# Attention: reciprocal row sums stored to DRAM, read back spread over feature rows, and multiplied into the PV output

## What is computed

```python
# q, k, v: (4, 8, 576, 64); block-causal mask in blocks of 64
scores = scale * q @ k.T
scores = where(block_i >= block_j, scores, -1e9)
attn = exp(scores - max(scores))
attn = attn / (sum(attn) + 1e-9)
out = attn @ v            # -> x (2304, 512), into the gated FFN and the experts
```

## Time and profile before

| | us |
|---|---|
| median of 3 runs (lowest, highest) | 1021.81 (1020.45, 1022.78) |
| profiled execution, its own time | 1020.62 |
| its span, first to last instruction | 1018.8 |
| attention, last PV's end in the span | 245.9 |
| TensorE busy in the span | 947.3 (93%) |
| VectorE busy in the span | 386.7 (38%) |
| mean granted TensorE clock | 0.970 |

### The profile page before, as it was taken

One profiled execution on the slowest core, in us unless ns is written; L12 is line 12 of the kernel. 1 busy time (PEld: TensorE's weight loads), 2 busy tenths in 40 slices (PEclk: granted clock), 3 DMA queues, 4 the chain that ended last, 5 costly groups with the idle time before them and its releaser, 6 DMA issues.

```text
span 1018.8 us, 15358 instructions
## 1 busy us (share of the span) xinstructions
PE 947.3 (93%) x5050; PEld 783.1 (77%) x5051; DVE 386.7 (38%) x962; ACT 341.1 (33%) x774; POOL 244.9 (24%) x241
## 2 busy tenths in 40 slices
PE   6898889988999999999999999999578998999995
PEld 3554545556999999999999999999457887888884
DVE  6878777784221120120111011011654444225421
ACT  4656666664222111211211211211254344125310
POOL 2122122121121111111111111111163545215511
PEclk9999999998999999999999999999679999999998
DMA  4234434331211010010010000000265538115310
GB/s 124 70 104 124 124 89 124 112 120 56 83 44 41 32 32 1 32 32 1 32 32 1 32 1 1 32 1 1 112 225 179 202 127 268 41 51 206 118 41 29
DMA packets 57313, 78.28 MB, mean 77 GB/s; under 512 B 22703, under 2 KB 34991, under 8 KB 57264
## 3 DMA queue, kind: packets, MB, share of 16 engines
q1 hardware_dynamic: 51504, 62.42, 19.7%
q0 software_dynamic: 3360, 10.49, 3.0%
q10 hardware_dynamic: 2400, 4.72, 1.2%
HBM read 63.46 MB, written 14.68 MB: 77 GB/s over the span
## 4 chain that ended last, share of the span: by engine, by line
PE 82%; DVE 7%; issue 6%; POOL 2%; DMA 2%; ACT 0%; SPq 0%; POOLq 0%; DVEq 0%; ACTq 0%
PE bank L1153 21%; PE bank L1155 21%; PE bank L1154 21%; PE bank L1084 6%; PE bank L1121 5%; PE bank L1103 3%; DVE prob L814 3%; PE bank L1290 2%; PE bank L1212 1%; DVE nmax L833 1%; DMA stage<-in_we 1%; POOL ew1l L365 1%; PE bank L1203 1%; PE bank L1264 1%; DVE pt L311 1%
## 5 line engine op out<-in xcount | busy, mean ns | idle before, releaser
L1153 PE MATMUL bank<-xh,w1h 128*128 128x384 f32 x576 | 196.0, 340 | 0.0
L1155 PE MATMUL bank<-xh,w1l 128*128 128x384 f32 x576 | 193.2, 335 | 0.0
L1154 PE MATMUL bank<-xl,w1h 128*128 128x384 f32 x576 | 193.1, 335 | 0.0
L885 DVE TENSOR_TENSOR hraw<-sig,bank 128x384 f32<-128x384 f32 x72 | 39.9, 555 | 353.9 <-ACT sig L722 353.9
L547 POOL TENSOR_TENSOR hl<-hraw,hh 128x384 fp32r<-128x384 f32 x72 | 77.2, 1073 | 401.2 <-ACT hh L693 401.2
L722 ACT ACTIVATE sig<-bank 128x384 f32<-128x384 f32 x72 | 35.4, 492 | 262.1 <-PE bank L1155 262.1
L1084 PE MATMUL bank<-kt,qbd 128*128 128x512 f32 (+7 forms) x320 | 115.8, 456 | 6.7 <-DVE kt L796 6.7
L1153 PEld LDWEIGHTS bank<-xh,w1h 128*128 128x128 f32 x576 | 108.2, 188 | 1.8
L1154 PEld LDWEIGHTS bank<-xl,w1h 128*128 128x128 f32 x576 | 108.3, 188 | 1.7
L1155 PEld LDWEIGHTS bank<-xh,w1l 128*128 128x128 f32 x576 | 108.1, 188 | 0.0
L656 ACT ACTIVATE prob<-bank,nmax 128x576 f32<-128x576 f32 (+2 forms) x144 | 76.1, 529 | 79.0 <-DVE nmax L833 77.0
(11 more groups left out here) (150 smaller groups left out, 1427.4 us busy)
## 6 DMA issues: line engine op xcount, KB each, us to landing
stage<-in_we SPq DMA_DIRECT2D x56, 512.0 KB, 4.4
w1raw<-in_w SPq DMA_DIRECT2D x8, 768.0 KB, 4.6
kt<-in_kT SPq DMA_DIRECT2D x16, 288.0 KB, 3.4
qbd<-in_qT SPq DMA_DIRECT2D x32, 144.0 KB, 4.0
xt_scratch<-xo SPq DMA_DIRECT2D x16, 288.0 KB, 2.1
xraw<-xt_scratch SPq DMA_DIRECT2D x6, 768.0 KB, 4.6
y_scratch<-yrow ACTq DMA_DIRECT2D x6, 768.0 KB, 3.5
vt<-in_v SPq DMA_DIRECT2D x16, 256.0 KB, 2.8
```

Source lines behind the costliest of these rows:

```text
L885: dve.tensor_tensor(hraw[:, f % 2, :], sig[:, f % 2, :], val_ps, ALU.mult).then_inc(hraw_done, 1)
L1153: pe.matmul(out_, wh, ah, start=first, stop=False, skip_group_check=True)
L1154: pe.matmul(out_, wh, al, start=False, stop=False, skip_group_check=True)
L1155: return pe.matmul(out_, wl, ah, start=False, stop=last, skip_group_check=True)
```

## The change

The probabilities stay unnormalised. The PV output has features on the partitions and queries along the free axis, so a query's factor must stand in all 64 feature rows of its head. The reciprocal sums of a pair, 128 rows of 9 values, are stored to a DRAM scratch `rinv_scratch` and read back, each head's 576 values into 64 partitions of `rwide`. `o_out` moves from ScalarE to VectorE and becomes a product of `rwide` and PSUM bank 3. The tiles in `prob` are kept for a whole pair, padded to multiples of 128 with zeros that are written once, and every transpose is 128 wide. `pt` holds for each key tile and head one contiguous run of queries. Units 3, 5, 6 and 8 go from ScalarE to VectorE, units 7 and 9 the other way. The w1 cast goes from ScalarE to GpSimd.

```diff
+    PT_STEP = 2 * S - P
+    rinv_dram = nc.dram_tensor("rinv_scratch", (2, 2, BLK, NB), F32, kind="Internal").ap()
-        prob = sb(s1, "prob", [P, SLOTS, S])
+        prob = sb(s1, "prob", [P, P * sum(i // 2 + 1 for i in range(NB))])
-        pt = [sb(s1, f"pt{i}", [P, KT_N, NB, P]) for i in range(2)]
+        pt = [sb(s1, f"pt{i}", [P, PT_STEP * (KT_N - 1) + 2 * S]) for i in range(2)]
+        rwide = sb(s1, "rwide", [P, BLK, NB])
-        BY_ACT = {1, 3, 5, 6, 8}
+        BY_ACT = {1, 7, 9}
+        RSUM_STEP, O_STEP = 2, 8
...
# evac_pT: one copy per unit
+            copy(bass.AP(tensor=rows.tensor, offset=rows.offset + PT_STEP * t0 + BLK * i,
+                         ap=[rows.ap[0], [PT_STEP, t1 - t0], [S, 2], [1, BLK]]),
+                 pT_psum(u)[:, 0:(t1 - t0) * P].rearrange("p (t h q) -> p t h q", h=2, q=BLK)).then_inc(done, 1)
...
# SyncE
+            def rinv_spread(g, par):
+                sp.wait_ge(rinv_done, g + 1)
+                sp.dma_start(rinv_dram[par].rearrange("h q i -> (h q) i"), rinv[:, par, :]).then_inc(rinv_stored, 16)
+                sp.wait_ge(rinv_stored, 16 * (g + 1))
+                if not (isinstance(g, int) and g == 0):
+                    sp.wait_ge(xo_done, g)
+                for h in range(2):
+                    sp.dma_start(rwide[64 * h:64 * h + 64].rearrange("d q i -> d (q i)"),
+                                 rinv_dram[par, h:h + 1].rearrange("a q i -> a (q i)").to_broadcast([64, S])
+                                 ).then_inc(rwide_loaded, 16)
...
                 if p >= 2:
+                    rinv_spread(g - 2, p % 2)
                     o_store(b, p - 2)
                 elif not isinstance(b, int):
+                    rinv_spread(g - 2, p % 2)
                     o_store(b - 1, p + 2)
                 if p % 2 == 1:
-                        sp.wait_ge(w1_high, W1_PARTS * k)
                         sp.wait_ge(w1_low, k)
...
             xload(0, PPB)
+            rinv_spread(NPAIR - 2, 0)
             o_store(BATCH - 1, PPB - 2)
+            rinv_spread(NPAIR - 1, 1)
             o_store(BATCH - 1, PPB - 1)
...
# GpSimd
+            def w1_split(k):
+                pool.wait_ge(w1_loaded, 16 * (k + 1))
+                pool.tensor_copy(w1h[...], w1raw[:]).then_inc(w1_high, 1)
+                pool.wait_ge(w1_high, k + 1)
                 pool.tensor_tensor(w1l[...], w1raw[:], w1h[...], ALU.subtract).then_inc(w1_low, 1)
...
# ScalarE: exponential
-                    if not (start and i < SLOTS):
-                        act.wait_ge(pT_done, NU * g + i - SLOTS + (2 if i >= SLOTS else 1))
+                    if not start:
+                        act.wait_ge(pT_done, NU * (g - 1) + i + 2)
...
# VectorE
+            def recips(g, par):
+                dve.wait_ge(exp_done, NB * (g + 1))
+                dve.tensor_scalar(rsum1[:], rsum[:, par, :], 1e-9, None, ALU.add).then_inc(rsum1_done, 1)
+                dve.wait_ge(rsum1_done, g + 1)
+                if not (isinstance(g, int) and g < 2):
+                    dve.wait_ge(rinv_stored, 16 * (g - 1))
+                dve.reciprocal(rinv[:, par, :], rsum1[:]).then_inc(rinv_done, 1)
+
+            def o_out(g, par):
+                dve.wait_ge(pv_done, g + 1)
+                dve.wait_ge(rwide_loaded, 32 * (g + 1))
+                if not (isinstance(g, int) and g < 2):
+                    dve.wait_ge(xo_stored[par], 8 * (g - par))
+                for half, i0, i1 in ((0, 0, 5), (1, 5, NB)):
+                    last = dve.tensor_tensor(
+                        xo[par][:, BLK * i0:BLK * i1].rearrange("p (i q) -> p i q", q=BLK),
+                        rwide[:, :, i0:i1].rearrange("p q i -> p i q"),
+                        bank[3][:, half, 0:BLK * (i1 - i0)].rearrange("p (i q) -> p i q", q=BLK), ALU.mult)
+                last.then_inc(xo_done, 1)
...
+                    if i == RSUM_STEP and not start:
+                        recips(g - 1, (p - 1) % 2)
                     if i >= LAG:
                         after_unit(g, p, i - LAG)
                     elif not start:
                         after_unit(g - 1, p - 1, i + NB - LAG)
-                    if not (start and i < 2):
-                        norm(n - 2, (i - 2) % NB, (s - 2) % SLOTS)
-                    if not (start and i < 1):
-                        denominator(n - 1, (s - 1) % SLOTS)
+                    if i == O_STEP and not start:
+                        o_out(g - 1, (p - 1) % 2)
...
# TensorE: turn waits for the exponential and turns 128 columns each time
-                pe.wait_ge(norm_done, NB * g + j + 1)
+                pe.wait_ge(exp_done, NB * g + j + 1)
+                        last = pe.transpose(pT_psum(u)[:, (t - t0) * P:(t - t0 + 1) * P],
+                                            prob[:, prob_at[j] + P * t:prob_at[j] + P * t + P], ident[:])
# pv
+                            last = pe.matmul(oT_at(h, a, e), vt[p % 2][0:K, j, 64 * h:64 * h + 64],
+                                             pt[p % 2][0:K, PT_STEP * j + S * h + a:PT_STEP * j + S * h + e],
```

More of the change, by code:

```diff
@@ L103, in bass_attention_ffn_moe @@
         vt = [sb(s1, f"vt{i}", [P, KT_N, P]) for i in range(2)]
-        prob = sb(s1, "prob", [P, SLOTS, S])
-        pt = [sb(s1, f"pt{i}", [P, KT_N, NB, P]) for i in range(2)]
+        prob = sb(s1, "prob", [P, P * sum(i // 2 + 1 for i in range(NB))])
+        pt = [sb(s1, f"pt{i}", [P, PT_STEP * (KT_N - 1) + 2 * S]) for i in range(2)]
         xo = [sb(s1, f"xo{i}", [P, S]) for i in range(2)]
[L107 to L110, removed]
+        nmax = sb(s1, "nmax", [P, NB])
+        rsum = sb(s1, "rsum", [P, 2, NB])
+        rsum1 = sb(s1, "rsum1", [P, NB])
+        rinv = sb(s1, "rinv", [P, 2, NB])
+        rwide = sb(s1, "rwide", [P, BLK, NB])
         s1.close()
@@ L284, in scores_at, with oT_at @@
             return bank[o // 2][:].rearrange("p a n -> p (a n)")[:, 0:S]
+        O_CUT = 5 * BLK
+        def oT_at(h, a, e):
+            half = a // O_CUT
+            return bank[3][64 * h:64 * h + 64, half, a - half * O_CUT:e - half * O_CUT]
         def pT_psum(u):
             return bank[2][:, u % 2, :]
[L289 to L294, removed]
+        prob_at = {}
+        for j in range(NB):
+            prob_at[j] = sum(P * tiles_of(x) for x in ORDER[:j])
         LAG, PE_LAG = 3, 4
-        W1_STEP = [4, 5, 6]
-        W1_PARTS = len(W1_STEP)
+        W1_STEP = 4
         PV_STEP = {4: [0], 5: [1], 6: [2], 7: [3, 4]}
-        O_STEP = 8
+        RSUM_STEP, O_STEP = 2, 8
         def evac_pT(copy, p, j, u, t0, t1, done):
             i = ORDER[j]
[L307 to L315, removed]
+            rows = pt[p % 2][:]
+            copy(bass.AP(tensor=rows.tensor, offset=rows.offset + PT_STEP * t0 + BLK * i,
+                         ap=[rows.ap[0], [PT_STEP, t1 - t0], [S, 2], [1, BLK]]),
+                 pT_psum(u)[:, 0:(t1 - t0) * P].rearrange("p (t h q) -> p t h q", h=2, q=BLK)).then_inc(done, 1)
         def gv_psum(f):
@@ L636, in after_unit @@
                         evac_pT(act.copy, p, j, u, t0, t1, pT_out_a)
[L638 to L645, removed]
             def pair(b, p):
@@ L661, in pair @@
                         after_unit(g - 1, p - 1, i + NB - LAG)
[L662 to L669, removed]
             for p in range(PPB):
@@ L684, in _ @@
             xhigh(0, 0)
-            o_out(NPAIR - 1, 1)
             act.wait_ge(scores_done, NB * NPAIR)
@@ L797, in _ @@
             q_zeros(1)
[L798 to L815, removed]
+            for j in range(NB):
+                if ORDER[j] % 2 == 0:
+                    dve.memset(prob[:, prob_at[j] + width(j):prob_at[j] + width(j) + BLK], 0.0)
+            def recips(g, par):
[16 more added lines that the diff above has]
+                last.then_inc(xo_done, 1)
             def after_unit(g, p, j):
@@ L864, in _ @@
             xlow(0, 0)
+            o_out(NPAIR - 1, 1)
             def yT_evac(i, m, last=False):
@@ L1087, in turn, with out_by @@
             def turn(g, p, j):
-                s = (NB * p + j) % SLOTS
-                start = isinstance(g, int) and g == 0
-                pe.wait_ge(norm_done, NB * g + j + 1)
+                pe.wait_ge(exp_done, NB * g + j + 1)
                 for u, t0, t1 in units_of(j):
-                    before_u, g0 = (u - 2, g) if u >= 2 else (u - 2 + NU, g - 1)
-                    if not (start and u < 2):
-                        if before_u in BY_ACT:
-                            pe.wait_ge(pT_out_a, AU * g0 + units_a[before_u + 1])
-                        else:
-                            pe.wait_ge(pT_out_v, VU * g0 + units_v[before_u + 1])
+                    out_by(u - 2 if u >= 2 else u - 2 + NU, g if u >= 2 else g - 1)
                     apart(pe)
                     for t in range(t0, t1):
-                        w = min(P, width(j) - P * t)
-                        last = pe.transpose(pT_psum(u)[0:w, (t - t0) * P:(t - t0 + 1) * P],
```

(20 more changed lines are left out.)

40 lines of the change are left out of this document (17 added, 23 removed).

## The result

The change made the kernel slower: 1101.2 us median of 4 runs (1099.6 to 1102.6) against 1022.1 (4 runs). The ratio is 1.078, 95% interval 1.0755 to 1.0796. The forecast was 1078 us with a range of 1052 to 1115.

A forecast was written before the change was run, and what follows sets the result against it. TensorE's pace bounds attention, a VectorE chain close behind. Periods +51 us, pair 15 and late rwide(14) -2, clock +8: 1020.6 + 57 = 1078 us, range 1052 to 1115.

The forecast's parts named there:

- The round trip is exposed: SyncE's reciprocal store and rwide reload start only after PV ends; rwide lands at +6.9 us, bounds 6.2 to 10.0.
- The chain to scores(3): From rwide's landing through o_out, the 576-wide maximum and exponential: scores(3) at +9.9 us, previously +4.4.
- Edits priced at nothing: Padded transposes, PV from runs, evacuations moved between ScalarE and VectorE, w1 cast on GpSimd, start memsets: no cost taken.
- rival 1: Attention stage: DMA round trip covered, under 3.3 us; period 13.7 us, total 1007 us, faster; 6 in 100.
- The collisions don't return: VectorE against GpSimd's subtraction: a product with only one SBUF input doesn't contend; pair 15 gains 2.7 us.
- kt in time: Next kt load and GpSimd scaling: ready at +17.9 us, wanted at 18.1+1.0, 1.2 us to spare.
- The period without a clock fall: Attention stage, one head pair: clean base 13.04 us plus 5.1 us of lag gives 18.1 us.
- The clock: TensorE's clock falling after idle gaps: 10 more falls at 0.8 us, +8 us; bounds 0 and 24.
- Rival 4: TensorE's clock: every gap brings a full fall on busy columns, +16 us on the forecast, 1094 us; 8 in 100.
- rival 3: Slow small DMA transfers of reciprocals: rwide lands at 10 us, total 1121 us; 12 in 100 for over 8.5.
- the forecast's own case: Attention stage: lag of 4 to 6.5 us a period, range 1058 to 1098 us; 68 in 100.

The follow-up runs named there:

- early spread: Changed kernel with SyncE storing and reloading the reciprocals before its wait for the end of PV instead of behind the vt loads; 1008.6 us, ratio 0.987.
- late product: Changed kernel with VectorE's product at step 3 of pair g+2, not step 8 of pair g+1, and w1raw loaded before the xo store; 1033.7 us, ratio 1.012.
- the spread early and the product dense: Changed kernel with reciprocals stored and reloaded before the PV wait, and rwide read as consecutive elements (output no longer attention's); 1004.4 us, ratio 0.982.

## Why the prediction was right, and where it was off

- **The round trip is exposed.** Right, step by step. Against the zero at 213.66: store issued +1.30 (predicted 1.3), first rwide issue +3.65 (3.6), second at 217.84, +4.18 (4.2), landed +7.02 (6.9). The early spread shows that it is the cause and the late product that the queue behind the product is its price.
- **The chain to scores(3).** Right: +9.86 (9.9). Within it 1.15 us pass from the product's start to that of the maximum instead of 0.9, because of the stride that was taken at nothing (the dense ones take 0.48 and 0.42 us); the hand-overs came out shorter.
- **Edits priced at nothing.** Right within what shows; the cast on GpSimd takes 1.5 us, inside its bounds. With the spread early and the product dense the period is 13.54 us, where rival 1 had 13.7.
- **The collisions don't return.** Right; no VectorE instruction of the changed kernel is stretched so, though GpSimd now has the cast as well.
- **kt in time.** Right in the changed kernel: none of TensorE's waits names it. After the gap shown its scaling ends at 231.94, +18.3 where +17.9 was predicted; in a period of 18.1 us that would have left 0.8 us, and the longer period left more. It did become late when the product was moved.
- **The period without a clock fall.** Right: 18.1 us predicted, 18.26 measured in the one period (20.00 to 38.26) whose work all ran at the higher level; the clock fell only in the idle time at its end (mean 0.97).
- **The clock: the step that failed.** The prediction took 10 more falls at 0.8 us each, +8, with 24 as the upper bound, and gave 8 in 100 to a full fall in every gap. The count was nearly right. All 14 gaps brought a fall, and 13 of these weigh on the 14 periods; all 13 had to be priced, as the periods that they are added to were built from one without a fall. The price was not: each cost 2.0 us. Scores(3) to scores(5) take 5.0 to 5.4 us behind the 13 gaps, with a mean of 5.27 (5.39 behind the one shown), and 3.26 with the early spread (160.98 to 164.24). Thirteen times 2.0 is 26 us, so the upper bound was too low as well. The falls were sized after those beside the collisions, where TensorE idled for 1.6 to 2.1 us and the clock was low for 3.4 us. Behind a gap of 5.4 to 6.4 us the low stretch is longer: by the 283.6 us above, with their mean of 0.84, 0.16 x 2 x 283.6 = 91 us were at the lower level, 6.5 us a period, part in the gap and part on work. Filling the gap took 27 us of the whole execution back.

The sum with the measured terms: 18.26 x 14 = 256, + 26 for the clock = 282, measured 283.6; the rest was not taken apart. The forecast of 1078 less its 8 for the clock, plus 30 (283.6 less the 253.4 of 14 periods of 18.1), is 1100 us. Rival 4 is thus what happened on top of the forecast's own mechanism, at a higher price than it was given. The result lies 3 us above the range that the forecast's own case was given, and inside the whole one. That is owed in part to the room left above for rival 3, slow transfers, which didn't come: the forecast with the clock's bound alone reaches 1094 us.

## What to carry to other kernels

Find the place of a new DMA in its in-order queue before pricing its duration: here the data was ready some 10 us early, and the store stood behind a wait for something else. Price a wait by what is queued behind it, and count a recurring idle time on TensorE twice, once as idle time and once as the slower clock on the work after it. And look at the old kernel's stretched instructions first: cutting one GpSimd instruction into twelve gave the 2% that the rework was worth at its best.

## What the runs showed that was not expected

- With idle times of 5.4 to 6.4 us once per 20 us, TensorE's granted clock fell each time, and the 5.4 us behind the gap shown had a mean of 0.55. With idle times of 1.3 to 1.4 us once per 14 us (early spread) it never fell in the 14 periods. In the kernel before, with 1.6 to 2.1 us beside each of seven collisions, it fell after three of them. The Trainium skill describes such an oscillation for waits between bursts of work (TensorE: Matmul & The Clock Gate, "HAM oscillation — how this bites in real kernels"); the trace agrees.
- A store of 128 rows of 36 bytes lands in 2.1 us (median) behind the vt loads, in 3.6 us behind the kt and qbd loads (early spread), and in 1.4 us as the second of two in a row. That the loads ahead make the difference is inferred from their order in the queue.
- Reading 64 times one DRAM row of 2304 bytes into 64 partitions is no slower than the other loads of 144 KB: 2.9 us, where qbd's take 4.1.
- VectorE's product with one operand in steps of 36 bytes: 1.92 ns an element; dense: 0.98.
